# Sparse attention and MoE on one core: the transposes of x ahead of those of the hidden activations

## The reference

```python
scores = scale * np.matmul(q, k.transpose(0, 1, 3, 2))
kth = np.partition(scores, -top_k, axis=-1)[..., -top_k:-top_k + 1]
scores = np.where(scores >= kth, scores, -1000000000.0)
...
return np.matmul(attn, v).astype(np.float32)
...
logits = x @ w_gate
noise_scale = np.log1p(np.exp(x @ w_noise))
noisy_logits = logits + noise_scale * noise
top2 = np.argpartition(-noisy_logits, 2, axis=1)[:, :2]
...
h = np.maximum(x[mask] @ w1[e], 0.0)
out[mask] += top2_w[mask, k, None] * (h @ w2[e])
```

## Time and profile before

| | us |
|---|---|
| median of three runs | 1321.51 (1318.83 to 1322.28) |
| the profiled execution | 1320.2 |
| its span, first to last instruction | 1318.5 |
| mean granted TensorE clock in it | 0.81 of full speed |
| TensorE busy | 1172.4 (89%) |
| VectorE busy | 919.6 (70%) |
| GpSimd busy | 740.1 (56%) |
| ScalarE busy | 588.8 (45%) |

### The profile page before, as it was taken

How to read it: one execution, slowest core, us unless ns; L and a number is a source line. 1 busy time by engine, 2 the same in 40 slices (tenths; PEclk the granted TensorE clock), 3 DMA queues, 4 the chain that set the end, 5 groups by cost and what they waited for, 6 DMA issues and landing times.

```text
span 1318.5 us, 20171 instructions
## 1 busy us (share of the span) xinstructions
PE 1172.4 (89%) x5919; PEld 1002.7 (76%) x5920; DVE 919.6 (70%) x1790; ACT 588.8 (45%) x1249; POOL 740.1 (56%) x600
## 2 busy tenths in 40 slices
PE   4899888789898988888889479999999999999997
PEld 3788777678787877777778468878788887888886
DVE  6999999999999999999997763334242424241221
ACT  3555555656655656556554332424242424242221
POOL 4877877778777877787773023334343433342221
PEclk7655776877666667777875589999999999999999
DMA  7502210221122102210200045342433334212120
GB/s 235 165 10 54 55 33 23 54 54 28 28 54 55 37 19 55 54 37 19 54 19 6 4 168 185 110 145 108 135 112 125 126 117 148 90 59 62 54 65 1
DMA packets 78047, 97.63 MB, mean 74 GB/s; under 512 B 47839, under 2 KB 47839, under 8 KB 77986
## 3 DMA queue, kind: packets, MB, share of 16 engines
q1 hardware_dynamic: 67346, 66.12, 16.5%
q0 software_dynamic: 10320, 30.16, 7.0%
q10 hardware_dynamic: 320, 0.59, 0.2%
HBM read 79.80 MB, written 20.71 MB: 76 GB/s over the span
## 4 chain that ended last, share of the span: by engine, by line
DVE 54%; PE 31%; DMA 10%; issue 2%; POOL 1%; ACT 0%; POOLq 0%; DVEq 0%; SPq 0%
DVE work L720 23%; DVE top L726 21%; PE ps_o L1124 14%; PE ps_h L1098 12%; DVE top L712 7%; DMA out<-y_sb,out_rows 4%; DMA prev<-out,out_rows 3%; DMA xin<-x_dram,tile_rows 2%; PE ps_s L1109 2%; PE ps_x L1081 1%; PE ps_o L1032 1%; POOL out_rows L488 1%; DVE y_sb L917 1%; PE ps_h L969 0%; DMA q_raw<-q_t 0%
## 5 line engine op out<-in xcount | busy, mean ns | idle before, releaser
L1032 PE MATMUL ps_o<-vA,pT 128*128 128x65 f32 (+3 forms) x1600 | 305.2, 348 | 31.1 <-ACT pT L594 30.8
L1032 PEld LDWEIGHTS ps_o<-vA,pT 128*128 128x128 f32 (+3 forms) x1600 | 268.3, 250 | 79.8 <-ACT pT L594 63.0
L450 POOL TENSOR_SCALAR probs<-scores,top 128x576 f32<-128x576 f32 x142 | 244.5, 1722 | 140.2 <-DVE top L726 77.0
L726 DVE MAX8 top<-work 128x8 f32<-128x576 f32 x432 | 305.0, 748 | 0.0
L1124 PE MATMUL ps_o<-W,hh 128*128 x688 | 224.0, 397 | 5.0 <-DVE hl L902 5.0
L1098 PE MATMUL ps_h<-W,xh 128*128 (+1 forms) x688 | 224.6, 398 | 1.4 <-DVE xl L881 1.4
L720 DVE MATCH_REPLACE8 work<-top,work 128x576 f32<-128x576 f32 x288 | 211.9, 744 | 0.0
L454 POOL TENSOR_TENSOR probs<-probs,expd 128x576 f32<-128x576 f32 x142 | 199.7, 1407 | 11.8
L917 DVE SCALAR_TENSOR_TENSOR y_sb<-ps_o,slot_weight,prev 128x512 f32<-128x512 f32 x43 | 32.3, 751 | 221.4 <-PE ps_o L1124 116.4
L1007 PE MATMUL ps_p<-ident,probs 128*128 128x128 f32 x576 | 130.4, 368 | 62.2 <-POOL probs L454 62.0
L951 PE MATMUL ps_s<-split 128*128 128x288 f32 x632 | 170.2, 415 | 11.6 <-DVE split L766 9.4
(11 more groups left out here) (146 smaller groups left out, 1642.9 us busy)
## 6 DMA issues: line engine op xcount, KB each, us to landing
raw<-w SPq DMA_DIRECT2D x16, 2048.0 KB
q_raw<-q_t SPq DMA_DIRECT2D x64, 144.0 KB, 2.9
k_raw<-k_t SPq DMA_DIRECT2D x60, 144.0 KB, 2.9
out<-zeros SPq DMA_DIRECT2D x18, 256.0 KB
vA<-v SPq DMA_DIRECT2D x32, 128.0 KB, 2.4
x_dram<-o_fin SPq DMA_DIRECT2D x32, 128.0 KB, 2.2
xin<-x_dram,tile_rows POOLq DMA_INDIRECT x43
prev<-out,out_rows POOLq DMA_INDIRECT x43
```

The lines of the kernel that those rows point to most:

```text
L450: nc.gpsimd.tensor_scalar(probs[:, s % PRING, :], scores[:, s % RING, :], top[:, s % RING, ROUNDS - 1, 7:8], None, ALU.is_ge).then_inc(mas ...
L726: nc.vector.max(top[:, r, n + 1, :], work[:, a, :])\
L1032: mm = nc.tensor.matmul(ps_o[a:z, 0:HD + 1], pT[0:rows, s % 2, c * P + a:c * P + z], vA[u][0:rows, h, c, :], start=(c == 0), stop=(c == KB))
```

## The change

PE's step begins with turn_x(n + 2), ahead of turn_h(n); it stood between hidden_of(n + 1) and results_of(n) before. No other queue and no semaphore is touched.

```diff
                 e = expert_of(n)
                 if exists(n, 1):
                     e_next = expert_of(n + 1)
+                if exists(n, 2):
+                    turn_x(n + 2, u)
                 turn_h(n)
                 if exists(n, 1):
                     hidden_of(n + 1, e_next)
-
-                if exists(n, 2):
-                    turn_x(n + 2, u)
                 results_of(n, e)
```

## The result

| | before | changed |
|---|---|---|
| median of five runs, us | 1321.51 | 1363.5 (1360.57 to 1366.97) |
| ratio, 95% interval | | 1.0324 (1.0308 to 1.034) |
| span of the profiled execution, us | 1318.5 | 1365.3 |
| PE's waits for xin in MoE | 3.4 us in 5 | 38.4 us in 10 |
| PE's waits for hl in MoE | 5.0 us in 6 | 1.2 us in 1 |

The medians differ by 42.0 us; 46.5 was forecast (1368 less 1321.5).

The account below looks back on a forecast made before the run. PE was taken to bound the MoE phase, losing only by waiting for x. Terms 31.8 + 2.2 + 4.7 + 3.5 + 1.0 + 3.4 = 46.6 us gave 1368 us; own range 1360 to 1376, widened to 1354 to 1384.

Parts of the forecast that it names:

- second stalls: PE's wait for the second late gather at each weight-loading opening: 2.7 us, of which 1.0 stays after a clock drop.
- tile 13: First late gather of x at tile 10's opening: lands about 921.6 but due at 916.4, stalling PE 5.1 us.
- tile 4: Its gather, at the first opening (tile 0), lands at 809.0 but is due at 804.27: 4.7 us.
- tile 33: Its gather, at the last opening (tile 30, no load), lands at 1173.5 but is due at 1169.99: 3.5 us.
- tile 40: Its gather follows a late scatter of tile 36, landing 1257.1 against 1256.1 due: 1.0 us.
- Ordinary steps: MoE steps away from openings: stay at 12.3 us without a wait, x landing with 1.6 us to spare.
- due time: When PE needs x landed: 6.36 us earlier in the new order, with turn_h(n) and hidden(n+1) behind that wait.
- rival d: Gathers held by turn_x would each leave 6.4 us earlier, removing 3.4 us of waits: 1318; chance 0.04.
- The openings with loads: Tiles 5, 10, 15, 20, 25: each 6.36 us net of old stalls plus 0.44 for later weight loads.
- Rival (c): Read of prev slips ahead of the weight load; an opening costs about 3 us, not 6.8: 1348; chance 0.10.
- a fall: PE's clock dropping to half behind long stalls: 1.7 us each, counted uncovered at two tiles, 3.4 us.
- Rival (a): Clock also falls at second stalls or stays low for microseconds: 8.5 to 14 us more, 1377 to 1383; chance 0.12.

Follow-up runs that it names:

- Experiment 1: Against the changed kernel, turn_x(n+2) put behind turn_h(n), still ahead of hidden(n+1): 1354.19 us, ratio 1.0266 to the kernel before.
- 2: Changed order, with GpSimd gathering x one tile further ahead: 1315.13 us, ratio 0.9973 to the kernel before.
- experiment 10: Changed order, with gather(n+4) issued directly behind scatter(n), ahead of the read of prev for tile n+1: 1325.01 us, ratio 1.0026 to the kernel before.
- experiment 4: Changed order, with each later load of weights cut to one partition of 128: 1331.52 us, ratio 1.01 to the kernel before.
- experiment 9: Changed order, with 40 idle transposes ahead of turn_x's wait in the step behind an opening: 1366.41 us, ratio 1.0358 to the kernel before.
- 5: Order of before, with each later load of weights cut to one partition of 128: 1310.52 us, ratio 0.993 to the kernel before.
- 7: Changed order, with three GpSimd memsets of 128 x 1024 in front of each gather inside the loop: 1393.02 us, ratio 1.0553 to the kernel before.

## Why the prediction was right, and where it was off

**The mechanism held.** PE waits for xin at the places forecast, but 38.4 us in 10 waits, where 40 to 48 in about 13 were forecast, since three second stalls are absent. By place: 5.1 us forecast at tile 13 and 6.3 measured, 4.7 and 4.5 at tile 4, 3.5 and 4.0 at tile 33, 1.0 and 1.6 at tile 40. Ordinary steps have no wait. Experiment 1 shows that the loss follows the due time, 2 that it vanishes with an earlier gather, 10 that the gather's place behind prev in GpSimd's queue is most of what makes it late. That the buffer is released earlier (rival d) gave nothing: GpSimd's waits name y, as before.

**The openings with loads: 34.0 us forecast, 29.9 measured.** Three of five cost 7.1 us on average in place of 6.8, two only 4.1 and 4.4. Rival (c), to which I gave one in ten for all five, happened at those two. Opening of tile 20, GpSimd and VectorE in order of time, first in the kernel before:
```profile
1035.06 4.49 DVE L848 TENSOR_TENSOR W<-raw,W 128x2048 f32 x2 [1.76 <-ACT W L649]
...
1035.36 2.04 POOL L488 COPY out_rows<-table 128x1 uint32 x1 [1.54 <-DMA out<-y_sb,out_rows]
1037.67 2.81 POOL L490 DMA_INDIRECT prev<-out,out_rows  x1 [0.27 <-POOL out_rows L488]
```
and in the changed one:
```profile
1066.04 0.18 POOL L488 COPY out_rows<-table 128x1 uint32 x1 [1.55 <-DMA out<-y_sb,out_rows]
1066.72 2.64 POOL L490 DMA_INDIRECT prev<-out,out_rows  x1 [0.51 <-POOL out_rows L488]
1069.37 1.32 POOL L477 COPY tile_rows<-table 128x1 uint32 x1
...
1066.15 4.50 DVE L848 TENSOR_TENSOR W<-raw,W 128x2048 f32 x2 [1.75 <-ACT W L649]
```
The split began 0.3 us ahead of the copy and now begins 0.1 us behind it, as it waits for hh, which comes 0.44 us later. So the copy takes 0.18 us, and prev goes out 0.6 us behind the beginning of the split, not 2.6. The load followed at 1070.82, so prev was 4.1 us ahead of it, not 2.05. From the scatter to the end of the gather's issue it is 8.5 us (1063.47 to 1071.96) and 11.3 at tile 10 (922.95 to 934.26), the same two lengths as without loads in experiment 4. What sets tile 20 apart is that its scatter lands sooner: GpSimd waits 1.55 us for it, and 1.88 at tile 10. That is 0.3 of the 2.8 us; the other 2.5 come from the order of copy and split, load or no load. How much of the saving beyond that comes from prev being in before the load is not shown.

**The clock.** I sized a fall at 1.7 us, too little for most of them. Behind the stall at tile 13 turn_x, turn_h and hidden took 1.11 + 1.71 + 6.81 = 9.6 us against 0.44 + 0.87 + 5.49 = 6.8, 2.8 us; at tile 23 it was 1.9. An estimate from the granted clock: work at 0.50 takes twice as long, so a fall costs half of the time that PE then works at 0.50. Behind the stall at tile 13 that was from 939.61 to about 945.2, which gives 2.8, at tile 23 from 1078.15 to about 1081.7, which gives 1.8. The second stalls, forecast at 2.7 us with 1.0 left, were 0.5 us at two openings and absent at three; so the error was covered there, and shows in the last opening (6.5 against 5.2). That the openings of tiles 5, 10 and 15 came to 7.3, 7.3 and 6.6 us against 6.8 is thus partly luck: at tile 13 the first stall was 1.2 us longer than forecast, and the clock cost about what the second stall was to have cost. Rival (a), a second fall at the second stalls, did not happen in the changed kernel; it did in experiment 9, where nothing ate them up.

**The ordinary step: 0 forecast.** The 20 that belong to no stall became 0.01 to 0.08 us shorter, 0.9 us together. From turn_h of tile 40 to that of tile 41 it is 0.5 us less, since the last turn_x now stands ahead of both.

**The sum** of 46.6 us set against 42.0 in the medians: the two cheap openings took 5.1 us off it, the ordinary steps 1.2 and the first opening 0.3, while the three dear openings, the last one and tile 40 added 0.8, 1.3 and 0.6. That leaves 42.7. The last terms nearly cancel, which is luck; and that the spans differ by 46.8, as forecast, is chance, by the 4.0 us of the phase's start.

## What to carry to other kernels

A step that is moved forward in a strict queue also moves forward the due time of what it waits for: add up the chain that produces it, from the instruction that releases it, and compare its spare with the distance moved, once for an ordinary pass and once for each special pass, where the spare was already used up. Where a wait hangs on something two passes back, a shortage shows in every other pass and costs half. And look for the cheaper cure in the producing queue: here the gather of x stood behind a read that waits for a write, and splits of weights that begin 0.2 to 0.7 us before a tiny copy hold up the whole of GpSimd's queue.

## What the runs showed of the hardware

- A copy of 128 x 1 elements on GpSimd takes 0.18 to 0.21 us. In the fourteen traces each of the 83 such copies of the MoE phase that began while a subtraction of 128 x 2048 ran on VectorE took 1.0 to 2.2 us, and ended 0.05 us behind the end of that subtraction. Of those that began 0.01 to 0.04 us ahead of one, 14 took 2.35 us and the others 0.2.
- Issuing an indirect DMA takes 1.0 us. Where such a subtraction was running when it began, it took 1.9 to 3.1 us in 210 of 214 cases. No transfer of weights is needed for either (experiments 4 and 5).
- Waits of PE of 1.0 to 2.0 us inside a full stream left the granted clock at 1.00 in experiments 7 and 9; waits of 2.8 and 3.3 us in experiment 9, and all of 2.2 us and more in experiment 7, were followed by 0.50. In experiment 10 waits of 2.01 us (up to 939.63) and 2.14 (up to 1004.53) were not, one of 2.06 (up to 873.28) was. In attention the fall at 679 came behind a stretch with 1.1 us of idle time.
- From issue to landing the gathers of x in the changed kernel and in experiment 10 took 3.2 to 4.2 us by themselves, and 7.1 to 8.1 us beside a load of 2 MB (from tile 4 on).
- A copy of one microsecond on ScalarE that nothing uses, ahead of the splits, made the old order 0.63% faster.
